# A new written-out order for five engine queues in a fused attention, gated MLP and mixer kernel

## The reference

```python
# attention: 8 heads of 64, each token sees itself and the 63 before it
scores = q @ k^T / 8;  masked to 0 <= i - j < 64;  softmax;  x = attn @ v          # (4, 576, 512)
# gated MLP
h = relu(x @ w_in);  u, v = h[..., :512], h[..., 512:]
v_n = (v - mean(v)) / sqrt(var(v) + 1e-6)
x = (u * (w_spatial @ v_n + b_spatial)) @ w_out
# mixer
u = x + (relu(x^T @ w_tok1) @ w_tok2)^T                                             # 576 -> 256 -> 576
out = u + relu(u @ w_ch1) @ w_ch2                                                   # 512 -> 1536 -> 512
```

## Time and profile before

| | us |
|---|---|
| median of 3 runs | 689.59 (687.06 to 689.68) |
| the profiled execution's own time | 687.06 |
| its span in the profile | 685.2 |
| TensorE busy in the span | 669.4 (98%) |
| VectorE, ScalarE, GpSimd busy | 322.3, 228.3, 150.6 |
| DMA engines, mean busy share of queue 1 | 29.2% |

### The profile page before, as it was taken

One profiled execution on the slowest core, in us unless ns is written; L12 is line 12 of the kernel. 1 busy time (PEld: TensorE's weight loads), 2 busy tenths in 40 slices (PEclk: granted clock), 3 DMA queues, 4 the chain that ended last, 5 costly groups with the idle time before them and its releaser, 6 DMA issues.

```text
span 685.2 us, 11477 instructions
## 1 busy us (share of the span) xinstructions
PE 669.4 (98%) x4133; PEld 620.0 (90%) x4133; DVE 322.3 (47%) x893; ACT 228.3 (33%) x642; POOL 150.6 (22%) x237
## 2 busy tenths in 40 slices
PE   5999999999999999999999989999999999999998
PEld 4898999999998899988999879999999999999996
DVE  4888967687666776766463411221221221221212
ACT  4865356434463335633347011121111111111110
POOL 3652427412143311342168300000000000000000
PEclk9999999999999999999999999999999999999999
DMA  9847015570036600006541540400300300400101
GB/s 248 212 66 166 2 35 102 94 150 5 17 68 129 122 16 17 15 10 192 155 149 59 121 156 1 139 0 1 138 0 0 138 0 0 139 0 1 47 0 47
DMA packets 139554, 50.66 MB, mean 74 GB/s; under 512 B 124144, under 2 KB 127792, under 8 KB 139504
## 3 DMA queue, kind: packets, MB, share of 16 engines
q1 hardware_dynamic: 139504, 50.00, 29.2%
...
## 4 chain that ended last, share of the span: by engine, by line
PE 92%; ACT 2%; SPq 2%; DMA 2%; DVE 1%; issue 1%; POOL 0%; DVEq 0%; POOLq 0%; ACTq 0%
PE ps L1124 67%; PE ps L1220 12%; PE ps L1164 4%; PE ps L1189 4%; PE ps L1174 2%; SPq L558 1%; PE ps L1283 1%; ACT att L721 1%; DMA uy<-u_scratch 1%; DMA u_scratch<-uy 1%; PE ps L1143 1%; DVE att L908 0%; ACT att L701 0%; DVE att L1112 0%; ACT xT L731 0%
## 5 line engine op out<-in xcount | busy, mean ns | idle before, releaser
L1124 PE MATMUL ps<-arena 128*128 128x288 f32 (+3 forms) x2064 | 353.3, 325 | 3.4 <-DVE att_r L1048 2.5
L1124 PEld LDWEIGHTS ps<-arena 128*128 128x128 f32 (+1 forms) x2064 | 323.4, 186 | 22.0 <-DVE att_r L1048 3.0
L1124 PE MATMUL ps<-arena,att_r 128*128 128x512 f32 x648 | 161.1, 393 | 0.0
L1048 DVE SCALAR_TENSOR_TENSOR att_r<-ps,att_r 128x384 fp32r<-128x384 f32 x72 | 40.0, 557 | 223.3 <-ACT att_r L811 223.3
L1124 PEld LDWEIGHTS ps<-arena,att_r 128*128 128x128 f32 x648 | 120.6, 188 | 22.0
L811 ACT ACTIVATE att_r<-ps 128x384 fp32r<-128x384 f32 x72 | 35.3, 492 | 250.6 <-PE ps L1124 250.6
L1220 PE MATMUL ps<-arena 128*128 128x288 f32 (+1 forms) x560 | 89.6, 316 | 0.0
L1220 PEld LDWEIGHTS ps<-arena 128*128 128x128 f32 x560 | 80.3, 188 | 3.9
L639 POOL TENSOR_SCALAR att<-att,rinv 128x128 f32<-128x128 f32 x144 | 56.8, 415 | 113.7 <-DVE rinv L919 113.6
L721 ACT ACTIVATE att<-att,nmax 128x128 f32<-128x128 f32 x144 | 55.9, 390 | 15.0 <-DVE nmax L908 14.8
L1189 PE MATMUL ps<-att 128*128 128x128 f32 x288 | 38.1, 276 | 1.2 <-issue 0.8
...
## 6 DMA issues: line engine op xcount, KB each, us to landing
...
```

Of the source, the lines that this page charges most:

```text
L1048: dve.scalar_tensor_tensor(out=h3[:, j % RING, 1, :], in0=ps[:, 6 + j % 2, 0:CK], scalar=0.0, in1=h3[:, j % RING, 0, :].bitcast(F32), op0= ...
L1124: ins = pe.matmul(dst, w[a], x[c], start=first and n == 0, stop=last and n == 2, skip_group_check=True)
```

## The change

Only the lists of names change: the same items, each once, in another order on TensorE, ScalarE, VectorE, GpSimd and SyncE. Waits and banks are derived from the lists as before. The lists of which the prediction speaks (the others are reordered in the same way):

```diff
     PROLOGUE_PE = (
-        "Q0 K0 Q1 S0 S1 K1 K2 S2 Q2 T0 S3 V0 T1 S4 V1 T2 S5 w0 w1 T3 V2 V3 T4 v0 T5 V4 V5 Q3 + K3 v1 Z4 S6 S7 + "
-        "v2 + S8 w2 u00 + T6 u10 + V6 T7 u20 w3 V7 T8 + u30 + V8 w4 v3 w5 + v4 + u01 + u11 + u21 + u31 +").split()
+        "Q0 K0 Q1 S0 K1 S1 S2 K2 S3 Q2 T0 V0 S4 T1 S5 V1 T2 T3 V2 V3 T4 v0 T5 V4 V5 Q3 + K3 v1 + Z4 S6 S7 v2 S8 "
+        "w0 + u00 + u10 + T6 u20 T7 V6 w1 + T8 V7 u30 V8 w2 + v3 w3 w4 + v4 + u01 w5 + u11 + u21 + u31 +").split()
     LOOP_PE = (
-        "g00 + g10 + S0 S1 g20 S2 + g30 + g01 T0 S3 S4 T1 + g11 + g21 + g31 + y00 + y10 + y20 V0 V1 + y30 + T2 S5 "
-        "T3 S6 V2 y01 + y11 + y21 + y31 + t0 T4 t1 V3 t2 S7 S8 t3 T5 V4 a0 a1 v0 T6 t4 V5 a2 a3 a4 + T7 V6 b00 "
-        "b10 b20 b30 b01 b11 v1 + b21 T8 V7 V8 b31 v2 + v3 + v4 + u00 + u10 + u20 + u30 + u01 + u11 + u21 + u31 +").split()
+        "g00 S0 S1 + g10 + g20 + g30 + g01 + g11 + S2 T0 S3 T1 g21 + g31 V0 S4 S5 + y00 + y10 + T2 S6 V1 V2 y20 + "
+        "y30 + y01 + t0 T3 t1 T4 y11 + y21 + y31 + V3 S7 t2 T5 V4 t3 S8 t4 T6 V5 a0 a1 a2 a3 T7 a4 V6 V7 v0 + b00 "
+        "T8 b10 b20 V8 b30 v1 + b01 b11 b21 v2 + b31 v3 + v4 + u00 + u10 + u20 + u30 + u01 + u11 + u21 + u31 +").split()
     EPILOGUE_PE = (
-        "g00 + g10 + g20 + g30 + g01 + g11 + g21 + g31 + y00 + y10 + y20 + y30 + y01 + y11 + y21 t0 t1 + y31 + a0 "
-        "t2 t3 a1 t4 a2 a3 a4 H0 H1 b00 b10 b20 b30 b01 b11 b21 b31").split()
+        "g00 + g10 + g20 + g30 + g01 + g11 + g21 + g31 + y00 + y10 + y20 + y30 + y01 + y11 + t0 t1 y21 + y31 + a0 "
+        "t2 a1 t3 t4 a2 a3 a4 H0 H1 b00 b10 b20 b30 b01 b11 b21 b31").split()
     PROLOGUE_ACT = (
-        "qe0 qe1 e0 e1 qe2 e2 o0 e3 e4 o1 xh0 e5 o2 wh0 o3 xh1 o4 o5 xh2 qe3 vr0 ze4 wh1 e6 vh0 vr1 e7 wh2 e8 "
+        "qe0 qe1 e0 e1 qe2 e2 e3 o0 e4 o1 xh0 e5 o2 o3 xh1 o4 o5 qe3 xh2 vr0 vr1 ze4 e6 vh0 e7 e8 wh0 vr2 o6 uu00 "
...
     EPILOGUE_ACT = (
-        "gh00 gh10 wb0 wb1 gh20 wb2 gh30 gh01 gh11 yy00 gh21 wb3 gh31 wb4 wb5 yy10 yy20 yy30 yy01 wb6 yy11 th0 "
-        "wb7 yy21 th1 yy31 uf0 th2 wb8 th3 th4 wb9 ah0 wb10 ah1 wb11 H0 H1 wb12 wb13").split()
+        "gh00 gh10 gh20 wb0 gh30 wb1 gh01 wb2 gh11 wb3 yy00 gh21 wb4 gh31 yy10 wb5 yy20 wb6 yy30 yy01 th0 yy11 "
+        "th1 yy21 wb7 yy31 uf0 th2 wb8 th3 th4 ah0 ah1 wb9 H0 H1 wb10 wb11 wb12 wb13").split()
     PROLOGUE_DVE = (
-        "ke0 m0 m1 vo1 r0 ke1 ke2 r1 m2 c0 hv0 hv1 m3 r2 c1 m4 lv0 r3 c2 r4 m5 c3 xl0 r5 vo2 c4 hv2 hv3 c5 lv2 "
+        "ke0 m0 ke1 m1 r0 m2 ke2 vo1 r1 c0 m3 r2 hv0 hv1 lv0 m4 c1 r3 hv2 r4 m5 c2 c3 xl0 r5 vo2 c4 hv3 c5 lv2 "
...
     EPILOGUE_DVE = (
-        "sa00 sm00 sa10 sm10 gl00 sa20 sm20 gl10 sa30 sm30 gl20 gl30 sa01 sa11 sm01 sm11 gl01 sa21 sm21 gl11 sa31 "
-        "sm31 gl21 gl31 tl0 tl1 tl2 tl3 tl4 al0 al1 te00 te10 H0 te20 H1 te30 te01 te11 te21 te31 ut0 ut1 ut2 ut3").split()
+        "sa00 sm00 gl00 sa10 sa20 sm10 gl10 sa30 sm20 sm30 gl20 sa01 sm01 gl30 gl01 sa11 sm11 sa21 gl11 sa31 sm21 "
+        "sm31 gl21 gl31 tl0 tl1 tl2 tl3 tl4 al0 al1 te00 H0 te10 te20 te30 te01 te11 te21 te31 ut0 H1 ut1 ut2 ut3").split()
     ALL_SP = (
-        "lq00 lk00 lq01 lv00 lv01 lq02 lk01 lk02 lw00 lw02 lw06 lk03 lz04 lv02 lq03 lv03 lw01 lv04 lw04 lk10 lq10 "
-        "lv10 lw03 lv11 lv12 lw05 lq20 lv13 lv14 lk20 st00 st01 lv20 sr00 st02 st03 sr01 sr02 lv21 sr03 lv22 lv23 "
-        "lk30 lv24 lq30 st10 st11 sr10 lv30 st12 sr11 sr12 st13 sr13 lv31 lv32 lv33 lv34 wb40 wb41 wb42 st20 wb43 "
-        "st21 st22 st23 sr20 sr21 sr22 sr23 wb44 wb45 wb46 uf40 wb47 wb48 wb49 wb410 wb411 wb412 wb413 sr30 sr31 "
-        "st30 st31 st32 sr32 sr33 st33").split()
+        "lq00 lk00 lq01 lv00 lk01 lk02 lv01 lq02 lw00 lv02 lv03 lq03 lz04 lk03 lw01 lw06 lv04 lw02 lk10 lw04 lq10 "
+        "lv10 lw03 lw05 lv11 lv12 lv13 lk20 lv14 st00 st01 lv20 st02 sr00 lq20 lv21 st03 sr01 sr02 sr03 lv22 lv23 "
+        "lk30 lv24 lq30 st10 lv30 sr10 st11 st12 sr11 st13 sr12 lv31 sr13 lv32 lv33 lv34 wb40 wb41 st20 st21 wb42 "
+        "wb43 sr20 st22 wb44 st23 wb45 sr21 sr22 sr23 wb46 wb47 wb48 wb49 uf40 st30 wb410 wb411 st31 wb412 sr30 "
+        "wb413 sr31 sr32 st32 st33 sr33").split()
```

More of the change, by code:

```diff
@@ L64, in bass_attention_gmlp_mixer_kernel @@
-        "+").split()
+        "g00 + g10 + S0 S1 g20 + g30 + g01 + g11 + g21 + g31 S2 T0 S3 + y00 + y10 + y20 + y30 + y01 S4 V0 S5 T1 "
+        "t0 + y11 + T2 V1 t1 y21 + y31 + S6 T3 V2 a0 a1 t2 T4 V3 t3 S7 V4 t4 a2 a3 a4 T5 S8 T6 V5 v0 + V6 T7 b00 "
+        "b10 b20 b30 b01 b11 b21 b31 v1 V7 T8 + V8 v2 + v3 + v4 + u00 + u10 + u20 + u30 + u01 + u11 + u21 + u31 +").split()
     LOOP_PE = (
-        "g00 + g10 + S0 S1 g20 S2 + g30 + g01 T0 S3 S4 T1 + g11 + g21 + g31 + y00 + y10 + y20 V0 V1 + y30 + T2 S5 "
@@ L74, in bass_attention_gmlp_mixer_kernel @@
-        "uu00 vr2 o6 o7 wh3 xh3 uu10 uu20 uu30 o8 vh1 xh4 wh4 wh5 vh2 vr3 vr4 uu01 vh3 vh4 uu11 uu21 uu31").split()
+        "qe0 qe1 e0 e1 qe2 e2 e3 o0 e4 o1 xh0 e5 o2 o3 xh1 o4 o5 qe3 xh2 vr0 vr1 ze4 e6 vh0 e7 e8 wh0 vr2 o6 uu00 "
+        "uu10 uu20 vh1 o7 xh3 o8 wh1 uu30 xh4 wh2 wh3 wh4 vh2 vr3 vr4 wh5 uu01 vh3 vh4 uu11 uu21 uu31").split()
     FIRST_ACT = (
-        "gh00 e0 gh10 e1 gh20 gh30 gh01 gh11 gh21 e2 gh31 yy00 yy10 e3 yy20 yy30 e4 yy01 o0 yy11 o1 th0 yy21 yy31 "
-        "e5 th1 th2 o2 th3 e6 th4 o3 e7 ah0 ah1 o4 vr0 o5 e8 o6 vh0 vr1 o7 vr2 o8 vh1 vr3 vh2 vh3 uu00 vr4 uu10 "
@@ L78, in bass_attention_gmlp_mixer_kernel @@
-        "uu20 uu30 uu01 vh4 uu11 uu21 uu31").split()
+        "gh00 gh10 gh20 e0 gh30 e1 gh01 gh11 e2 yy00 yy10 gh21 gh31 yy20 yy30 o0 e3 yy01 th0 th1 o1 e4 yy11 yy21 "
+        "e5 o2 yy31 th2 e6 th3 th4 o3 e7 o4 ah0 ah1 o5 vr0 o6 e8 o7 vr1 vh0 o8 vr2 vh1 vh2 vr3 uu00 vr4 uu10 uu20 "
+        "vh3 vh4 uu30 uu01 uu11 uu21 uu31").split()
     LOOP_ACT = (
-        "gh00 e0 e1 gh10 gh20 gh30 e2 e3 gh01 e4 gh11 o0 o1 yy00 gh21 yy10 yy20 gh31 yy30 e5 yy01 yy11 e6 yy21 o2 "
-        "th0 yy31 th1 o3 th2 th3 e7 e8 o4 th4 o5 ah0 ah1 vr0 o6 vh0 vr1 o7 o8 vr2 vh1 vh2 vr3 uu00 vr4 uu10 uu20 "
@@ L82, in bass_attention_gmlp_mixer_kernel @@
-        "vh3 uu30 uu01 uu11 vh4 uu21 uu31").split()
+        "gh00 e0 gh10 e1 gh20 gh30 e2 e3 gh01 o0 e4 yy00 gh11 o1 gh21 o2 gh31 yy10 yy20 yy30 e5 yy01 th0 th1 yy11 "
+        "yy21 e6 yy31 o3 th2 o4 th3 th4 e7 e8 o5 ah0 ah1 o6 o7 vr0 o8 vr1 vh0 vh1 vr2 vh2 vr3 uu00 uu10 vr4 vh3 "
+        "uu20 vh4 uu30 uu01 uu11 uu21 uu31").split()
     EPILOGUE_ACT = (
-        "gh00 gh10 wb0 wb1 gh20 wb2 gh30 gh01 gh11 yy00 gh21 wb3 gh31 wb4 wb5 yy10 yy20 yy30 yy01 wb6 yy11 th0 "
-        "wb7 yy21 th1 yy31 uf0 th2 wb8 th3 th4 wb9 ah0 wb10 ah1 wb11 H0 H1 wb12 wb13").split()
+        "gh00 gh10 gh20 wb0 gh30 wb1 gh01 wb2 gh11 wb3 yy00 gh21 wb4 gh31 yy10 wb5 yy20 wb6 yy30 yy01 th0 yy11 "
@@ L86, in bass_attention_gmlp_mixer_kernel @@
+        "th1 yy21 wb7 yy31 uf0 th2 wb8 th3 th4 ah0 ah1 wb9 H0 H1 wb10 wb11 wb12 wb13").split()
     PROLOGUE_DVE = (
-        "ke0 m0 m1 vo1 r0 ke1 ke2 r1 m2 c0 hv0 hv1 m3 r2 c1 m4 lv0 r3 c2 r4 m5 c3 xl0 r5 vo2 c4 hv2 hv3 c5 lv2 "
-        "xl1 hu0 hu1 wl0 ke3 vs0 xl2 m6 vn0 hu2 m7 wl1 hu3 r6 vs1 m8 r7 vo3 c6 vl0 r8 wl2 c7 vn1 vo4 c8 vs2 xl3 "
-        "wl3 kt0 vn2 xl4 wl4 kt1 vl1 vl2 wl5 vs3 vs4 vn3 vn4 vl3 vl4").split()
+        "ke0 m0 ke1 m1 r0 m2 ke2 vo1 r1 c0 m3 r2 hv0 hv1 lv0 m4 c1 r3 hv2 r4 m5 c2 c3 xl0 r5 vo2 c4 hv3 c5 lv2 "
@@ L90, in bass_attention_gmlp_mixer_kernel @@
+        "xl1 vo3 hu0 hu1 hu2 ke3 vs0 xl2 m6 vn0 hu3 m7 r6 m8 vs1 r7 vl0 r8 wl0 c6 vs2 c7 vo4 vn1 c8 kt0 xl3 vl1 "
+        "wl1 vn2 xl4 wl2 kt1 wl3 vl2 wl4 vs3 vs4 vn3 wl5 vn4 vl3 vl4").split()
     FIRST_DVE = (
[4 rows of a table removed]
-        "kt0 ut2 vl3 vn4 ut3 kt1 vl4").split()
[4 rows of a table added]
+        "vs4 ut3 vn4 vl3 vl4 kt1").split()
     LOOP_DVE = (
[3 rows of a table removed]
-        "vo4 te11 c8 kt0 te21 te31 vs1 ut0 vs2 ut1 vn1 vn2 ut2 vl1 vl2 vs3 vn3 ut3 vs4 vl3 kt1 vn4 vl4").split()
[3 rows of a table added]
+        "vn0 te01 te11 te21 vn1 vl0 vl1 te31 ut0 vs2 ut1 vn2 vl2 vs3 vn3 vs4 ut2 ut3 vl3 vn4 vl4 kt1").split()
@@ L106, in bass_attention_gmlp_mixer_kernel @@
     FIRST_POOL = (
-        "la0 lo0 lo1 n0 lo2 lo3 n1 n2 n3 la1 la2 n4 n5 xh0 lb0 xl0 lb1 n6 n7 xh1 xl1 xh2 rs0 n8 xl2 xh3 xl3 rs1 "
+        "lo0 la0 n0 lo1 lo2 lo3 n1 n2 la1 n3 la2 n4 xh0 lb0 lb1 n5 xl0 n6 xh1 n7 xh2 xl1 rs0 n8 xl2 xh3 xl3 rs1 "
         "xh4 xl4 rs2 rs3 rs4").split()
     LOOP_POOL = (
-        "n0 n1 n2 n3 n4 n5 xh0 xh1 xl0 n6 n7 xh2 xl1 xl2 rs0 n8 xh3 xl3 xh4 xl4 rs1 rs2 rs3 rs4").split()
+        "n0 n1 n2 n3 n4 n5 xh0 n6 xl0 n7 n8 xh1 xh2 xl1 xl2 xh3 rs0 xh4 xl3 xl4 rs1 rs2 rs3 rs4").split()
     EPILOGUE_POOL = (
```

## The result

The changed kernel takes 691.84 us, the median of 19 runs (690.94 to 693.34); the kernel before, run beside it, 688.60 (19 runs, 685.44 to 691.83). The ratio is 1.0056, interval 1.0041 to 1.0070: slower by 0.56%, 3.8 us; the two medians are 3.2 us apart. That is at the 3.4 us which the prediction took as the bound of no change, and the interval does not say on which side. The executions of the kernel before form two groups, 685.4 to 687.1 and 688.5 to 691.8 (in the later sets of runs, which list the granted clock, the upper group has nearly always 0.995 to 0.998 and the lower 0.999 or 1.0), so its median moves with their mix: 688.60 here, 686.2 to 686.9 in the later sets. Numbers of different sets are therefore compared by their ratios to the kernel before, and to some 1.5 us. The prediction was 691.2, range 686.8 to 695.5.

The account below looks back on a forecast made before the run. The prediction took TensorE, busy 669.4 of 685.2 us, as the bound. Loops -0.7, prologue +0.2 and passage to the last stage +2.1 gave +1.6 on a median of 689.59: 691.2 us, range 686.8 to 695.5.

Parts of the forecast that it names:

- The loops: Loop rounds: TensorE's pause between V7 and V8 goes in two rounds, no new pauses; -0.7 us.
- The prologue: Prologue: an earlier start of v1 against more dense TensorE work; +0.2 us in sum.
- w0, w1 cost 0.9 in dense work: Prologue: w0 and w1, eight transposes, move from a pause to where none is; +0.9 us.
- v1 0.7 us earlier: Prologue: the new load and mask order lets ScalarE run exponents without gaps, so v1 starts 0.7 us earlier.
- 1.0 us to spare: Loop rounds: y01 needs gl31, which by the count of the queues is ready with 1.0 us to spare.
- (b) The door: Passage to the last stage: TensorE's 0.85 us wait for bank 3 goes, but this is worth nothing.
- (a) ScalarE behind wb13: Passage: ScalarE waits for the late load wb413, so hidden piece 4 starts at 393.3, not 390.12; by itself +3.2 us.
- (c) Chunk 1's input: Passage: this load follows all stores, which end later; hidden piece 8 starts at 411.7, +2.1 us.
- the passage: The way to the last stage, 381 to 410 us: largest term, +2.1 us, lower bound -1.6, upper +5.7.
- The stores hide the loads: Rival at the passage: DMA has room for the loads beside the stores; passage -1.6, total 687.5 us; chance 0.15.
- hidden pauses go: Rival at 34 to 381 us: unseen TensorE pauses shrink, -6, 685.3 us; chance 0.07 including a larger prologue gain.
- The queue runs no fuller: Rival at the passage: DMA share stays 0.82 with loads and stores mixed; passage +5.7, total 694.8 us; chance 0.22.

Follow-up runs that it names:

- e2: The kernel before with only the changed loop lists (FIRST and LOOP) and their share of SyncE's list; 686.97 us, ratio 0.9998.
- e1: The kernel before with only the changed prologue lists and their share of SyncE's list; 689.38 us, ratio 1.0030.
- e7: The changed kernel with VectorE's prologue list reordered, copies of the transposed probabilities moved ahead; 691.90 us, ratio 1.0074.
- e3: The kernel before with only the changed epilogue lists and their share of SyncE's list; 695.14 us, ratio 1.0112.
- e9: The changed kernel with TensorE filling its wait ahead of hidden piece 4 with 18 matmuls whose result is never read; 691.29 us, ratio 1.0076.
- e11: The kernel before with chunk 1's input load issued once the last batch's four `st` stores have landed, ahead of the rest loads; 684.68 us, ratio 0.9970.
- e12: Changed kernel with old prologue lists, w_ch loads ahead of last stores, GpSimd waiting for gl31, chunk 1's input load issued early; 683.08 us, ratio 0.9948.

## Why the prediction was right, and where it was not

The sign and the range hold, and the order of the size: +1.6 was forecast, +3.8 came by the ratio, +3.2 by the medians. That 691.84 lies so near to 691.2 is luck in part: the sum started from a median before of 689.6, and with 19 runs that is 688.60. By its steps, in the profiled executions:

- **The loops, -0.7.** Measured -0.68 between the first `g` of the first round and that of the epilogue, with no new pause; e2 has it alone. That T8, V7 and V8 had 0.37 us to give twice, and that LDWEIGHTS' 90% hid nothing more, was read correctly from the starts.
- **The prologue, +0.2.** Measured +1.42, and some 1.7 over the profiles: the term was mis-sized. The part "w0, w1 cost 0.9 in dense work" fits (v1 starts 0.45 late with w0 and w1 still to be done, `g` 1.42), but what I had against it, "v1 0.7 us earlier", is 0.45 later. I had followed ScalarE's exponents and not the two PSUM banks that T and V share: V1 needs c1, which stands behind m3, hv0, hv1, lv0 and m4, and o0, which stands behind e3; T2 then comes at 22.18 instead of 20.60. e1 shows the loss alone; e7 shows that moving VectorE's copies does not repair it. ScalarE's share in it is argued from e7's waits.
- **The epilogue's gate, no term at all.** Measured +1.52. I followed the queues of LOOP and cost the epilogue's moved `wb` items at nothing. The new ScalarE order feeds GpSimd from 344.45 on, in the middle of the gate; before, it was silent from 346.04 to 352.12. The "1.0 us to spare" for y01 was counted for the loops, where GpSimd has no such load. The trace of before held the hint: its own gl31, at 352.41 beside GpSimd's 352.12, took 1.88 us and not 0.46.
- **(b) The door, "worth nothing".** It went (-1.0), and 4.3 us of waiting stand behind it at piece 4, as the step says. e2, which has no stop there, does not test that: its piece 8 comes 1.0 sooner after the epilogue's `g` than before (74.6 and 75.6 us).
- **(a) ScalarE behind wb13.** Predicted: piece 4 at 393.3, with the segment's end where it was. That end came 2.27 us later (the last `b` item starts at 379.85, then at 382.12), so the forecast stands for 395.57; measured 395.71. The way there differs: the issue of wb413 came 2 us later still, at 389.08, as `sr30`'s four issues took 1.19 each in the full queue and not 0.55, and it was taken up 4.6 us after its issue and not 6.3. The bytes ahead of it took the time that was worked out, so the landing fits and the issue does not.
- **(c) Chunk 1's input at 411.7 as the later stop.** Wrong. It was issued at 403.27 and split at 408.92, ready before TensorE came; there is no wait at piece 8. By (a) alone piece 8 was due at 395.71 + 16.9 = 412.6; it came at 413.85. The 1.2 us between are the clock after the wait (piece 4 lasts 3.5 us from start to start and not 2.1), which the prediction did not have.
- **Sum.** From the last b item to piece 8 the passage costs +2.02 (29.71, then 31.73), against +2.1. That this fits is luck in part: (c) was 1 us too late and the clock's 1.4 missing.
- **The rivals.** "The stores hide the loads" and "hidden pauses go" are out. "The queue runs no fuller" is out too: the share in 382 to 396 is 1.04. Its 694.8 is near e3's 695.14, but by another cause, waits and clock.

The prediction cited the Trainium skill, "DMA: Bandwidth & Descriptors", for a semaphore's write landing behind all earlier writes of its engine. The four loads, issued at 381.7 to 389.1, were taken up at 386.12, 387.91, 389.98 and 393.63 by ScalarE, one behind the other and each behind the stores ahead of it, which agrees; that a load could not have passed the stores is not shown by it.

Open: what sets the prologue's pace item by item, what the slower four executions of e3 lose, why e9's set of runs does not show its profile's gain, and the remaining slow executions of e11 and e12.
